# Second router's logits from an early copy of seven experts' sum, the eighth expert's share added later

## What is computed

```python
# first mixture: x -> x1
for e in range(E):                      # 8 experts, D 512, F 1024
    for k in range(2):
        mask = top2[:, k] == e
        h = np.maximum(x[mask] @ w1[e], 0.0)
        out[mask] += top2_w[mask, k, None] * (h @ w2[e])
# second mixture, x is now x1
do_compute = x @ w_skip > 0
logits = x[do_compute] @ w_gate         # 8 columns
e_idx = np.argmax(logits, axis=1)
gate_w = softmax(logits)[e_idx]
out = x.copy(); out[do_compute] += gate_w * expert[e_idx](x[do_compute])
```

## Time and profile before

| what | value |
|---|---|
| median of 3 runs | 729.18 us (725.63 to 731.9) |
| profiled execution, its own time | 726.76 us |
| its span, first to last instruction | 724.9 us |
| TensorE busy | 653.6 us (90%) |
| VectorE busy | 375.6 us (52%) |
| ScalarE busy | 292.9 us (40%) |
| GpSimd busy | 205.8 us (28%) |
| DMA traffic | 116.16 MB |
| mean granted TensorE clock | 0.958 of full |

### The profile page before, as it was taken

How to read it: one execution, slowest core, us unless ns; L and a number is a source line. 1 busy time by engine, 2 the same in 40 slices (tenths; PEclk the granted TensorE clock), 3 DMA queues, 4 the chain that set the end, 5 groups by cost and what they waited for, 6 DMA issues and landing times.

```text
span 724.9 us, 13743 instructions
## 1 busy us (share of the span) xinstructions
PE 653.6 (90%) x4192; PEld 577.0 (80%) x4192; DVE 375.6 (52%) x731; ACT 292.9 (40%) x503; POOL 205.8 (28%) x227
## 2 busy tenths in 40 slices
PE   5786884699999999999999999999699998999992
PEld 4675773389999999999999999976478876777771
DVE  2684697736364546345463645402574576636621
ACT  2362673024343444343343534405065474644620
POOL 0537580130241506051332415030022232221321
PEclk9898997599999999999999999999799999999997
DMA  9999996026272735537192827357355678557221
GB/s 192 204 223 237 267 291 230 20 80 206 75 215 68 185 132 126 201 80 247 50 258 68 219 73 187 129 97 217 96 198 179 178 255 268 152 146 261 44 43 16
DMA packets 94867, 116.16 MB, mean 160 GB/s; under 512 B 55940, under 2 KB 56068, under 8 KB 94800
## 3 DMA queue, kind: packets, MB, share of 16 engines
q1 hardware_dynamic: 77264, 90.83, 41.5%
q0 software_dynamic: 10464, 23.81, 15.7%
q10 hardware_dynamic: 7072, 0.71, 0.8%
HBM read 100.01 MB, written 20.18 MB: 166 GB/s over the span
## 4 chain that ended last, share of the span: by engine, by line
PE 57%; DMA 20%; SPq 8%; issue 7%; DVE 4%; POOLq 1%; POOL 1%; ACT 1%; DVEq 0%; ACTq 0%
PE bank L797 20%; PE bank L791 20%; DMA out<-y_sb,ix_put 10%; DMA xg<-x_moe,ix_take 8%; SPq L502 6%; PE bank L648 3%; PE bank L780 2%; PE bank L769 2%; SPq L517 2%; PE bank L720 2%; PE bank L698 1%; PE bank L681 1%; PE bank L710 1%; PE bank L898 1%; PE bank L670 1%
## 5 line engine op out<-in xcount | busy, mean ns | idle before, releaser
L1462 DVE TENSOR_TENSOR w_lo<-stage,w_hi x120 | 141.5, 1221 | 19.3 <-ACT w_hi L1022 17.4
L1022 ACT CAST w_hi<-stage x120 | 119.6, 1047 | 9.5 <-PE bank L898 9.4
L797 PE MATMUL bank<-unit_hi,w_hi 128*128 128x416 f32 x256 | 92.6, 362 | 0.0
L791 PE MATMUL bank<-tok_hi,w_hi 128*128 128x416 f32 x256 | 90.4, 353 | 0.0
L797 PE MATMUL bank<-unit_lo,w_hi 128*128 128x416 f32 x256 | 90.1, 352 | 0.0
L797 PE MATMUL bank<-unit_hi,w_lo 128*128 128x416 f32 x256 | 89.8, 351 | 0.0
L791 PE MATMUL bank<-tok_hi,w_lo 128*128 128x416 f32 x256 | 89.8, 351 | 0.0
L1696 DVE SCALAR_TENSOR_TENSOR unit_lo<-bank,unit_hi 128x416 fp32r<-128x416 f32 x64 | 37.9, 592 | 96.6 <-ACT unit_hi L1108 80.7
L1108 ACT ACTIVATE unit_hi<-bank 128x416 fp32r<-128x416 f32 x64 | 33.1, 518 | 128.6 <-PE bank L791 116.3
L1310 POOL DMA_INDIRECT x_moe<-rows_out,ix_put x32 | 58.8, 1837 | 53.3 <-DVE rows_out L1685 46.0
L791 PE MATMUL bank<-tok_lo,w_hi 128*128 128x416 f32 x256 | 58.5, 349 | 0.0
(11 more groups left out here) (163 smaller groups left out, 1114.6 us busy)
## 6 DMA issues: line engine op xcount, KB each, us to landing
stage<-in_moe_w SPq DMA_DIRECT2D x128, 512.0 KB, 6.2
v_win<-in_v SPq DMA_DIRECT2D x24, 192.0 KB, 6.6
x_moe<-rows_out SPq DMA_DIRECT2D x12, 260.0 KB, 4.0
x_att<-x_sb POOLq DMA_DIRECT2D x12, 256.0 KB, 5.2
x_sb<-x_moe SPq DMA_DIRECT2D x12, 256.0 KB, 2.8
out<-x_moe SPq DMA_DIRECT2D x4, 768.0 KB, 8.9
late_raw<-in_v SPq DMA_DIRECT2D x6, 384.0 KB, 7.6
stage<-in_k SPq DMA_DIRECT2D x6, 256.0 KB, 6.7
```

The source lines that it names most:

```text
L791: last = eng.matmul(ps_unit[f % 2][:, 0:W], w, x, start=(i == 0), stop=(i == len(mine) - 1))
L797: last = eng.matmul(ps_out[chunk][:, 0:W], w[:, WC // 2 + f, chunk * P:(chunk + 1) * P], h[:, f % UNITS, :], start=(f == 0 and i == 0), st ...
L1022: eng.copy(piece(w_hi[n % SETS], j), stage[:, j, :]).then_inc(s_hi, 1)
L1462: eng.tensor_tensor(piece(w_lo[n % SETS], j), stage[:, j, :], piece(w_hi[n % SETS], j).bitcast(F32), ALU.subtract)\
```

## The change

`x_moe1` gets rows of 521 columns: 512 of x1 and 9 of logits. When seven experts' rows are scattered, the first 512 columns are copied to a new DRAM tensor `x_part`; the second router's tiles are loaded from that copy. In the last expert's round and the turning after it, TensorE multiplies each chunk of 128 output columns by the router's weights, summing over the chunks in a free place of a PSUM bank; VectorE scales the nine numbers by the gates, and they are scattered in the same rows as the output. After the last scatter they are loaded (`more_logit`) and added by VectorE to the router's result. The loads of tiles 9 to 11 stand behind that wait. The last `put` waits until the copy is through (`s_may_put`). Fillers: 24 and four times 4 become 20 and once 8; the 60 at the seam go. `x1_sb` now shares the place of `rows_in`. In the sync engine's queue the last four of the weight pieces loaded ahead move behind the copy.

```diff
+LOGITS = E + 1
-    x1_dram = nc.dram_tensor("x_moe1", (N, ROW), F32, kind="Internal").ap()
+    x1_dram = nc.dram_tensor("x_moe1", (N, D + LOGITS), F32, kind="Internal").ap()
+    part_dram = nc.dram_tensor("x_part", (N, D), F32, kind="Internal").ap()
+        ps_more = ps_out[0][:, W:W + PARTS * LOGITS]
-        XR = 4
+        XR = PARTS
+        x1_sb = rows_in[:, :, 0:D]
...
@@ sync engine @@
             for g in range(PIECES, ready):
+                if g == ready - PIECES // 2:
+                    land(0)
+                    eng.wait_ge(s_counted, 1)
+                    eng.reg_load(counts, todo_i[0:1, 0:E])
+                    eng.reg_mov(total, 0)
+                    for e in range(E - 1):
+                        eng.reg_add(total, total, counts[e])
+                    eng.wait_ge(round_sems["yfree"],
+                                eng.snap(total, min_val=0, max_val=E * ROUNDS) + 1)
+                    for rows in base_rows:
+                        eng.dma_start(part_dram[rows, :], x1_dram[rows, 0:D]).then_inc(s_part, 16)
                 load_piece(g)
                 land(AIR - 1)
-            land(0)
-            eng.wait_ge(s_m1done, 1)
+            eng.wait_ge(s_part, 16 * BASES)
+            eng.sem_inc(s_may_put, ROUNDS)
+            eng.reg_add(total, total, counts[E - 1])
+            eng.wait_ge(round_sems["xtp"],
+                        eng.snap(total, min_val=0, max_val=E * ROUNDS) * PARTS + (PARTS + 1))
             for t in range(NT):
                 if t >= XR:
                     eng.wait_ge(s_x1t, t - XR + 1)
-                eng.dma_start(x1_sb[:, t % XR, :], x1_dram[t * P:(t + 1) * P, 0:D])\
+                if t == NT - 3:
+                    eng.wait_ge(s_m1done, 1)
+                    for i, (t0, t1) in enumerate(GROUPS[1]):
+                        more = x1_dram[t0 * P:t1 * P, D:D + LOGITS]
+                        eng.dma_start(more_logit[:, t0:t1, :],
+                                      more.rearrange("(t p) e -> p t e", p=P)).then_inc(s_more[i], 16)
+                eng.dma_start(x1_sb[:, t % XR, :], part_dram[t * P:(t + 1) * P, :])\
                    .then_inc(s_x1[t % XR], 16)
+            land(0)
...
@@ TensorE @@
-                def turn_y(n, chunk):
+                def turn_y(n, chunk, logits=False):
...
+                    for t in range(PARTS if logits else 0):
+                        last = eng.matmul(ps_more[0:PART[t], t * LOGITS:(t + 1) * LOGITS],
+                                          out_t[:, PSTART[t]:PSTART[t] + PART[t]],
+                                          wgate2[:, (chunk - 1) % DK, :],
+                                          start=(chunk == 1 and t == 0),
+                                          stop=(chunk == 0), skip_group_check=True)
...
+                                if e == E - 1 and chunk == 0:
+                                    eng.wait_ge(S["ye"], n * DK + 2)
-                                    turn_y(n, chunk)
+                                    turn_y(n, chunk, logits=(e == E - 1))
...
-                keep_warm(24, ps_turn)
+                keep_warm(20, ps_turn)
                 for t in range(PARTS):
                     eng.wait_ge(s_take[t], 16)
                     turn_x(0, t, ps_out[t])
-                    keep_warm(4, ps_turn)
+                keep_warm(8, ps_turn)
+                eng.wait_ge(s_last_gates, 2)
...
-            keep_warm(60, ps_unit[0])
             eng.wait_ge(s_xt_idle, 1)
             for t in range(NT + 2):
                 if t < NT:
                     eng.wait_ge(s_x1[t % XR], 16 * (t // XR + 1))
+                    if t == 1:
+                        eng.wait_ge(s_xt_idle, 2)
...
@@ GpSimd: put(), and the loop over the experts @@
+                    eng.wait_ge(s_may_put, n + 1)
+                        if e < E - 1:
+                            eng.sem_inc(s_may_put, 1)
...
@@ VectorE: route(1, group) @@
-                    then(eng.tensor_copy(logit2[:, tiles].rearrange("p t e -> p (t e)"),
-                                         second_place(t0, t1)))
+                    eng.wait_ge(s_more[group_no[m, group] - 1], 16)
+                    then(eng.tensor_tensor(
+                        logit2[:, tiles], second_place(t0, t1).rearrange("p (t e) -> p t e", t=T),
+                        more_logit[:, tiles], ALU.add))
...
@@ VectorE: first_mixture @@
+                def logits(n, seen):
+                    eng.wait_ge(S["ytp"], n * DK + 1)
+                    eng.wait_ge(s_last_gates, seen + 2)
+                    for t in range(PARTS):
+                        rows = PART[t]
+                        last = eng.tensor_scalar(rows_out[0:rows, t, D:D + LOGITS],
+                                                 ps_more[0:rows, t * LOGITS:(t + 1) * LOGITS],
+                                                 gates_last[0:rows, t:t + 1], None, ALU.mult)
...
                             if f == 1:
+                                if e == E - 1:
+                                    logits(n, dn)
                                 columns(n, 0)
...
+                                if e == E - 1:
+                                    eng.tensor_copy(gates_last[:], gates_next[:, :, e])\
+                                       .then_inc(s_last_gates, 1)
...
+                eng.wait_ge(S["xte"], PARTS + 1)
+                eng.memset(ps_more, 0.0).then_inc(s_last_gates, 1)
...
-                columns(eng.snap(number, min_val=0, max_val=E * ROUNDS), 0)
+                eng.drain().then_inc(s_xt_idle, 1)
+                n = eng.snap(number, min_val=0, max_val=E * ROUNDS)
+                logits(n, eng.snap(counts[E - 1], min_val=0, max_val=ROUNDS))
+                columns(n, 0)
```

More of the change, by code:

```diff
@@ L194, in build @@
         gates_now = sb("gates_now", [P, PARTS])
+        gates_last = sb("gates_last", [P, PARTS])
         lane_h = sb("lane_h", [P, P], F16)
@@ L276, in build @@
         den = sb_in(routing, "den", [P, NT])
+        more_logit = sb_in(routing, "more_logit", [P, NT, LOGITS])
         gates = sb_in(routing, "gates", [P, NT, E])
@@ L289, in build @@
         gt_sb = sb_in(routing, "gt_sb", [E + 1, 2, P])
-        XR = 4
+        XR = PARTS
         second = ExitStack()
-        x1_sb = sb_in(second, "x1_sb", [P, XR, D])
         xt_b = [sb_in(second, f"xt_b{i}", [P, DK, P]) for i in range(2)]
@@ L297, in build @@
         xt_hi, xt_lo = [sb_in(routing, f"xt_{part}", [P, DK, P], F32R) for part in ("hi", "lo")]
-        xg = sb_in(routing, "xg", [P, ROW])
+        xg = sb_in(routing, "xg", [P, D + LOGITS])
         y_sb = sb_in(routing, "y_sb", [P, D])
@@ L308, in build @@
         out_t = sb_in(rounds, "out_t", [P, W])
-        rows_out = sb_in(rounds, "rows_out", [P, PARTS, ROW])
+        rows_out = sb_in(rounds, "rows_out", [P, PARTS, D + LOGITS])
         rounds.close()
+        x1_sb = rows_in[:, :, 0:D]
         zeros = rows_out[:, PARTS - 1, :]
@@ L367, in build @@
         s_xt_idle = sem("s_xt_idle")
+        s_part = sem("s_part")
+        s_may_put = sem("s_may_put")
+        s_last_gates = sem("s_last_gates")
+        s_more = [sem(f"s_more{i}") for i in range(2)]
         s_x1t = sem("s_x1t")
@@ L521, in _ @@
             flying = []
+            counts = [eng.alloc_register(f"sp_rounds{e}") for e in range(E)]
+            total = eng.alloc_register("sp_total")
             def land(most):
@@ L581, in _ @@
             ready = (E + SETS) * PIECES
+            base_rows = [slice(i * N // BASES, (i + 1) * N // BASES) for i in range(BASES)]
             for g in range(PIECES, ready):
+                if g == ready - PIECES // 2:
[9 more added lines that the diff above has]
+                        eng.dma_start(part_dram[rows, :], x1_dram[rows, 0:D]).then_inc(s_part, 16)
                 load_piece(g)
                 land(AIR - 1)
-            land(0)
-            eng.wait_ge(s_m1done, 1)
+            eng.wait_ge(s_part, 16 * BASES)
[3 more added lines that the diff above has]
+                        eng.snap(total, min_val=0, max_val=E * ROUNDS) * PARTS + (PARTS + 1))
             for t in range(NT):
@@ L591, in _ @@
                     eng.wait_ge(s_x1t, t - XR + 1)
-                eng.dma_start(x1_sb[:, t % XR, :], x1_dram[t * P:(t + 1) * P, 0:D])\
+                if t == NT - 3:
[5 more added lines that the diff above has]
+                eng.dma_start(x1_sb[:, t % XR, :], part_dram[t * P:(t + 1) * P, :])\
                    .then_inc(s_x1[t % XR], 16)
-            for i in range(BASES):
-                rows = slice(i * N // BASES, (i + 1) * N // BASES)
+            land(0)
+            for rows in base_rows:
                 eng.dma_start(out[rows, :], x1_dram[rows, 0:D]).then_inc(s_base, 16)
@@ L812, in one_round @@
                             if f == 1:
-                                turn_y(n, 0)
+                                turn_y(n, 0, logits=(e == E - 1))
                         if part == 0:
@@ L854, in first_mixture @@
                         one_round(e)
```

(9 more changed lines are left out.)

## The result

The changed kernel took 722.59 us (median of 20 executions), the one before 726.95 (20). The ratio is 0.9932, with a 95% interval from 0.9909 to 0.9955: 4.9 us faster (4.4 by the two medians), where I had forecast 9.0. Repeated twice on other occasions, it was 0.9966 [0.9936, 0.9996] and 0.9945 [0.9917, 0.9973]. The gain is real, about half of the forecast. The median 722.59 lies inside my range (713 to 728), but the gain is 0.7%, under the 1% to which I had given 0.62.

A forecast was written before the change was run, and what follows sets the result against it. TensorE holds 57% of the chain; the transition is bound by the last scatter, for which the whole router waits. Terms: -2.0 at the start, -7.0 at the seam, -9.0 in all, giving 719.4 us from the mean 728.4; range 713 to 728.

The forecast's parts named there:

- rival A: Second router: without fillers the clock halves for at least half the stretch, 732.7 us or 734.3 against the mean; chance 0.06.
- C: Seam: small logit rows take 7.9 us, tile 9 waits over 5 us, only 0.6 gained there, 725.8 us; chance 0.20.
- D: Round 8: the copy to x_part, over 12 us longer than allowed, holds the last scatter; chance 0.05.
- The start, "-2.0": Before the first mixture's products: twelve fewer fillers gain 2.0 us, bounds 0 and 2.8, the last gather being next late.
- The rounds, "3.2 us for four turnings": Round 8: logit matmuls in four output turnings add 3.2 us on TensorE; bounds for five turnings 3.0 to 5.2.
- The copy, "cost 0": Round 8: copying seven experts' sum finishes by 467, with 12 us of cover before the last scatter, costing 0.
- The seam, "-7.0": Between the mixtures: tile 9 starts at 495.3 instead of 502.34, 7.0 us earlier, logit work included.
- 485.31 plus (479.3 - 474.6) = 490.0: Seam: time when the wait for the last scatter ends, shifted from the old 485.31 by the later end of VectorE's scalings.
- The small rows, "add 1.5 us": Seam, tile 9's load: 1,536 logit rows of 36 bytes ahead of it add 1.5 us to its 3.04.
- Rival B: Second mixture: the odd row pitch slows gathers; one us more in each of 14 slots gives 733.4; chance 0.05.
- rival E: More gain: logit work 2.0 less, small rows free (1.5), 2.8 at the start, -13.3 in all, 715.1 us; chance 0.12.
- limit of 721.9: Whole kernel: time below which it counts as faster, about 1% or 7.3 us from no change; chance of faster 0.62.

The follow-up runs named there:

- old_start: Changed kernel with the fillers at the start of the first mixture as before (24, and 4 behind each part's turning): 724.12 us.
- no_logit_mm: Changed kernel without round 8's matmuls with the router's weights, so the eighth expert's logits are zero: rounds took 318.89 us; no whole time given.
- no_loads: Changed kernel without the five tile loads (tiles 4 to 8) beside the last scatters; router reads stale tiles; span 702.9 us (one execution), which means nothing.
- fill_tile9: Changed kernel with fourteen filler matmuls ahead of TensorE's wait for tile 9: 719.71 us.
- one_group: Changed kernel with late logit loads, fillers at tile 1 and rearranged at the start, one route of twelve tiles instead of two of six: 720.31 us, ratio 0.9916.
- combo_mid: Changed kernel with logit loads behind all tile loads, four fillers ahead of tile 1 and of the ranks, start fillers rearranged: 717.87 us, ratio 0.9912.
- before_521: Kernel before the change with only x_moe1's rows widened to 521 columns, the last zero and unused: ratio 1.0015 to the kernel before.
- tail_last: Changed kernel with the eighth expert's logit loads, and the wait ahead of them, moved behind all twelve tile loads: 720.33 us.
- ranks_later: Changed kernel with late logit loads, fillers at tile 1 and rearranged at the start, first group's ranks and exponentials one tile later: 718.00 us, ratio 0.9895.
- changed_again: Changed kernel with no edit, run again as a control: 722.56 us, ratio 0.9966 to the kernel before.
- changed_twice: Changed kernel with no edit, run once more as a control on another occasion: 722.80 us, ratio 0.9945 to the kernel before.

## Why the prediction was right, and where it was short

**The mechanism.** Right. The router no longer waits for the last scatter; its first transposes follow the last logit matmuls at once (479.01, after 478.35 and 0.74 us), it stands where I said, and its last wait is the logits' tail. No rival took over as a whole. The sign that I had put down for rival A did appear, a clock of 0.50 in the router, but for 3.5 to 6.8 us and not for half of its 28, and tile 9's wait stayed under the 5 us of C. D is excluded: the copy issued at 457.94 and the tile loads, which are queued behind the wait for it, at 474.39, 7 us before the first quarter of the last scatter was issued.

```profile
457.94 2.62 SPq L611 DMA_DIRECT2D x_part<-x_moe  x4
...
474.39 12.31 SPq L628 DMA_DIRECT2D rows_in<-x_part  x9
```

**The start, "-2.0".** Measured -1.2 by the profiles, -1.3 and -1.6 by old_start. I let the twelve fillers go at their price and named the last gather as next late, at the right place; I left out that TensorE's gaps between the gathers then lie bare, and that the clock can fall there. Eight fillers and the first products at the low level cost part of the gain in one profile of three.

**The rounds, "3.2 us for four turnings".** Measured 3.7 (no_logit_mm). The 0.80 us from the first router's tile was a little over the 0.73 on the chain; the 0.2 us that each group does to the product behind it was missing. The bounds (3.0 to 5.2 for five) held it: five cost 4.4.

**The copy, "cost 0".** Right: its cover was long enough, and the delayed weight pieces were used only in the second mixture. But they are landed before the router's tiles may load, and the sync engine had only 0.9 to 1.6 us to spare; in no_logit_mm it had none, and TensorE stood for tile 0.

**The seam, "-7.0", the step that failed.** Apart from the rounds, -6.7 in place of -10.2. In the three profiles of the changed kernel tile 9 starts 20.6 to 21.5 us after ScalarE's last copy, where the sum has it at 19.6 (495.3 less 475.7), and from there to the last logits it takes 8.1 to 9.3 us for 6.7 before: on average 1.4 and 2.2 us too little, 3.6 in all. Two terms are missing. First: "485.31 plus (479.3 - 474.6) = 490.0" moved the last scatter with its old landing time. The queue was empty then; now five tile loads run beside the scatters. I had priced these loads for themselves, and they were nearly free (the longest wait for one of them in the three profiles is 0.31 us, at tile 7). no_loads puts their company at 1.8 to 2.4 us; the 1.5 us for the small rows, 1.0 to 1.2 too much, hid part of it in the sum. Each transfer had been priced against its own deadline and none against the one on the path. Second: the low clock around tile 9, 1.4 to 2.7 us by fill_tile9. I had weighed a fall of the clock as rival A for the whole stretch, and dismissed short falls as lying inside the range; they belonged in the sum, because the earlier trace rows had shown the clock at 0.50 no later than 1.3 us after TensorE's last work at 509.7, and the stand that I had forecast was 2.4 us. Of the Trainium skill's rule that transposes don't count as busy for the clock gate (TensorE: Matmul & The Clock Gate, Part 4: PE-mode transpose), the router shows again what it showed before: in the profile after, the clock held 1.00 from tile 1 to tile 8 in this mix, and it came back to 1.00 at 503 in the middle of it. The rule alone does not decide here: each fall named in this text lies in a stand of TensorE or within 1.4 us behind one.

**The small rows, "add 1.5 us".** More than was needed: tile 9's load took 3.58 us behind them, 3.48 and 3.30 in the other two profiles (3.04 without), and rival C, with 7.9 us, did not happen. In time the result lies where C lies; by its place it is another thing.

**Rival B and the second mixture.** Its gathers landed with a median of 4.5 us, as before. Still the second mixture was longer in the changed kernel's profiles, 199.4 to 201.9 us against 198.0 and 198.7, and 203.8 in one_group; but combo_mid, which has the change too, had 198.31. before_521 gives the wider rows no measurable loss, and no experiment here explains the rest. I had no term for it. It stays open; with it, the difference between the sum of the profiles' parts (-1.8) and the times (-2.5 to -4.9).

**Readings and sums that were off and moved nothing.** The 57% of TensorE in the chain aren't the first mixture alone: its products and turnings have 44%, the rest is fillers, routers, attention and second mixture in small shares. The 8.3 us of VectorE's first route contained the 1.65 us wait named under tail_last. In rival E the "2.0 less" for the logit work has no source: my own bounds (3.0 for 4.0) give 1.0. And the limit of 721.9 is taken from the median of 729.18, my 719.4 from the mean of 728.4; from the mean it is 721.1.

## What to carry to other kernels

When a transfer is pulled out of a wait and put beside the work that the wait was for, price what it does to the transfer that is still on the path: here loads that nothing had to wait for made the last scatter 2 us late. Where one engine issues loads in the order of its program, put the load with the latest source last; moving two small loads behind three that needed nothing was worth 2.2 us by the times and 3.3 in the seam. And when a long filler is removed, list the stands that remain and their lengths: the stand of 3.3 to 3.7 us ahead of tile 9 cost its own length and another 1.4 to 2.7 us in clock. Filling a stand works where its length is known (fill_tile9) and did not where it varied (combo_mid's four fillers ahead of the ranks); queueing work that isn't waiting, as ranks_later did, took the stand away.

## What the runs showed that I had not expected

The clock fell with stands of quite different lengths, and at no fixed place: in the profile after it fell between 499.5 and 500, about a microsecond after work had resumed, and at 151.5, after two gaps of 0.49 and 0.68 us; in changed_again, changed_twice, combo_mid and tail_last it fell while TensorE still stood. tail_last lost the clock at tile 1's stand of 1.03 us, the profile after did not at one of 1.08; and with gaps of 0.41 and 0.68 us at its start, tail_last kept it there. Eight fillers of 512 columns took 2.11 us at the high level (changed_again) and 3.45 at the low one.

The version with ranks_later's edits beats both kernels: 0.9895 of the kernel before against 0.9945 of the changed kernel on the same chip, 1.0% for 0.5%, from the same idea. The intervals overlap (0.9857 to 0.9933 and 0.9917 to 0.9973); the seam, 33.23 for 38.00 us, says the same.
